# Second MLP product of nine blocks by seven sums, with the split first weights kept in DRAM

## The chip, the cores and the metric

One core of a Trainium2 chip. The metric is the device time of the whole program in microseconds (us). The granted TensorE clock was 1.00 in every stretch of the profile shown below.

## The reference

Attention with normalised queries and keys, then two MLPs of a model width of 768 and a hidden width of 3072, over 4 batches of 448 positions, all in fp32:

```python
x = attention(rmsnorm(q), rmsnorm(k), v)             # (4, 448, 768)
xn = (x - mean(x)) / sqrt(var(x) + 1e-06) * g_ln
x = x + maximum(xn @ w_ch1a, 0.0) @ w_ch2a           # first MLP
u = x + (x.transpose(0, 2, 1) @ U @ V).transpose(0, 2, 1)
out = u + maximum(u @ w_ch1b, 0.0) @ w_ch2b          # second MLP
```

## The kernel before

**Stages.** After the attention the MLP work is four stages `s`: stages 0 and 1 are the first MLP for the batches 0, 1 and 2, 3, stages 2 and 3 the second MLP. A stage has six blocks `j`. A block makes 512 hidden rows as two groups `g` (products of kind `G`, with `w1`), and then multiplies them with `w2` (products of kind `M`), adding to `acc`.

**Kind G.** A 2 by 2 block product made from seven products (`P1` to `P7`, order `ORDER`) of sums of inputs and of weights. The sums of the inputs (`in_hi`, `in_lo`) are made once for a stage, the sums of the weights once for a group by GpSimd (`weight_sum`, into `w_s1`, `w_s2`, or in place). VectorE puts the seven results together (`combine`), in the tiles `t_u2`, `t_c22`, `t_c12`, `t_c21`.

**Kind M.** Plain: 12 products a block (`OUTS`: six rows of output `d`, two halves), each for both batches and two chunks. After the second half VectorE adds two banks to `acc` (`gather`), twelve additions a block.

**Splitting.** Every operand is split into a high part in fp32r and a low part. ScalarE makes the high part (`weight_high`, `hidden_high`), VectorE subtracts to get the low one (`weight_low`, `hidden_low`), and TensorE makes three passes, high by high, high by low and low by high. So a `G` product is 3 chunks by 3 passes = 9 matmuls, an `M` product 2 x 2 x 3 = 12. A block has 14 x 9 + 12 x 12 = 270 matmuls, all 128x128 by 448 columns.

**Order.** `prods` is a list of all products. Every engine walks the same list, each at its own pace, and position `n` of the walk is product `n`. On VectorE a position is, in this order: a step of `mixing` where there is one, `weight_low` for the product 3 positions on, `hidden_low` or `make_low`, and last `combine` or `gather` of product `n`, which waits for that product. The split weights lie in a ring of 8 slots. A product's bank of PSUM (six of them) is given back when it has been read out. SyncE issues all DMAs, in the order of its own walk.

**Mixing.** In stages 1 and 2 twelve items of the step from the first to the second MLP (`U`, `V`) are run between products. An item begins every `MIX_STEP` = 22 positions. Its step for chunk `i` is: TensorE transposes at offset 4 + 3i, ScalarE `xs_hi` at 5 + 3i, VectorE `xs_lo` at 6 + 3i, and TensorE waits for that `xs_lo` at 7 + 3i. At offset 19 TensorE waits for what VectorE does at 18, and at 20 VectorE adds to `xa` twice.

Of the kernel before, what the change touches and what calls it, by code (L numbers as in the profile page):

```python
# [5 lines left out]
F32 = mybir.dt.float32  # L6
# [23 lines left out]
def mixer_kernel(nc, qkv, q_t, g_qk2, g_ln, u_lr, v_lr, w1, w2, out_t):  # L30
# [8 lines left out]
    STAGES = B  # L39
    assert D * 2 == P and KC == HC and NG == 2 * NJ and DC == 6 and B == 4  # L40
    xres = nc.dram_tensor("xres", (B, DC, P, S), F32).ap()
    xnrm = nc.dram_tensor("xnrm", (B, DC, P, S), F32).ap()


    prods = []
    for s in range(STAGES):
        for j in range(NJ):
            for g in (2 * j, 2 * j + 1):
                prods += [("G", s, g, k) for k in ORDER]
            prods += [("M", s, j, n) for n in range(len(OUTS))]  # L50
# [6 lines left out]
    def j_no(q):  # L57
        return prods[q][1] * NJ + prods[q][2]
# [5 lines left out]
    for q, (kind, s, n, k) in enumerate(prods):  # L64
# [3 lines left out]
        if kind == "M" and OUTS[k][1]:  # L68
            onto = number[kind, s, n, OUTS.index((OUTS[k][0], 0))]
        if onto is not None:  # L70
            banks[q] = banks[onto]
            before[q] = [onto]
        else:
            banks[q] = [free.pop(0) for _ in range(1 if kind == "G" else 2)]
            before[q] = [last_use.get(b) for b in banks[q]]
        if kind == "G" and k in LAST_IN_BANK or kind == "M" and OUTS[k][1]:
# [6 lines left out]
    for q in range(Q):  # L83
        kind, _, _, k = prods[q]
        if k == 0 or kind == "M" and k == 6:
            runs.append([])
        runs[-1].append(q)
        run_of.append(len(runs) - 1)
    high_at, low_at, sums_at, reload_at = {}, {}, {}, {}
    for r, run in enumerate(runs):  # L90
        for q in run:
            high_at.setdefault(q - 4, []).append(q)
            low_at.setdefault(q - 3, []).append(q)
        if prods[run[0]][0] == "G":
            for k, at in ((P5, -5), (P7, -5), (P6, -4), (P3, 0)):
                sums_at.setdefault(run[0] + at, []).append((r, k))
        reload_at.setdefault(run[-1] - 2, []).append(r)
    sum_no = {}
    for at in sorted(sums_at):
        for what in sums_at[at]:  # L100
            sum_no[what] = len(sum_no)
# [4 lines left out]
    def group_run_before(r):  # L106
        return next((n for n in range(r - 1, -1, -1) if prods[runs[n][0]][0] == "G"), None)

    RING = 8


    store_at = {}
    for s in range(STAGES):
        for d in range(DC):
            store_at[number["M", s, NJ - 1, OUTS.index((d, 1))] + 2] = s, d
# [32 lines left out]
    MIX_FROM, MIX_STEP, ITEMS = 4, 22, 2 * HC  # L148

    def mix_of(q):  # L150
# [3 lines left out]
        m, off = divmod(q - number["G", s, 0, 0] - MIX_FROM, MIX_STEP)  # L154
# [18 lines left out]
    with ExitStack() as ctx:  # L173
# [86 lines left out]
        w_in = [sem(f"w_in{i}") for i in range(2)]  # L260
        make_in = [[sem(f"make_in{c}_{n}") for n in range(4)] for c in range(HC)]
# [122 lines left out]
        def outs_done(s, j, d):  # L384
            return 12 * (s * NJ + j) + 2 * (d + 1)


        def read_out(eng, q, n=0):
            kind, s, j, k = prods[q]
            if kind == "M":  # L390
                eng.wait_ge(ev_done, outs_done(s, j, OUTS[k][0]) - 1 + n)
            elif k == P1:
                eng.wait_ge(p1_done, g_no(q) + 1)
            elif k == P2:
                eng.wait_ge(hlo_done, cut(g_no(q), C11))
            else:
                eng.wait_ge(comb_done, 5 * g_no(q) + COMB[k])


        def ended(q):  # L400
            return g_no(q) if 0 <= q < Q and prods[q][0] == "G" and prods[q][3] == P4 else None

        with nc.Block() as block:
            @block.sync
            def _(sp):
# [16 lines left out]
                def load_weights(r):  # L422
                    if r >= len(runs):
                        return
                    if r >= 2:
                        sp.wait_ge(wlo_done, runs[r - 2][-1] + 1)
                    kind, s, n, k = prods[runs[r][0]]
                    src = w1[s // 2, n].rearrange("p a c -> p (a c)") if kind == "G" else w2[s // 2, n, k // 6]
                    sp.dma_start(w_raw[r % 2][:].rearrange("p a c -> p (a c)"), src).then_inc(w_in[r % 2], 16)

                def load_made(s, c, n):
# [7 lines left out]
                    else:  # L439
# [6 lines left out]
                        if c == 2:  # L446
                            sp.wait_ge(hlo_done, 4 * NG * s)
# [34 lines left out]
                for what, n in seq:  # L482
# [17 lines left out]
                    if what != "step":  # L500
# [3 lines left out]
                        for r in reload_at.get(n, ()):  # L504
                            load_weights(r + 2)
# [759 lines left out]
```

## Time and profile before

| | |
|---|---|
| time, median of 3 runs | 1702.59 us (1702.48 to 1703.29) |
| time of the profiled execution | 1701.09 us, with a span of 1699.2 us |
| TensorE (PE) busy | 1660.1 us of the span, 98% |
| VectorE (DVE) busy | 1093.7 us, 64% |
| ScalarE (ACT) busy | 703.5 us, 41% |
| GpSimd (POOL) busy | 484.7 us, 29% |
| HBM traffic | 122.75 MB read, 24.77 MB written |

The span is cut into 40 equal slices in the profile. The first eight or so are attention; the MLP stages follow, from about 344 us to the end. A matmul's duration in the profile overlaps with that of the next one, so durations of matmuls are not added up. The lines (L772 and so on) are those of the kernel printed above.

### The profile page before, as it was taken

Reading aid. Unit: us, or ns where it says so; the run is one execution under the profiler, and the core shown is the slowest. Engines: PE = TensorE matmul, PEld = TensorE weight load, DVE = VectorE, ACT = ScalarE, POOL = GpSimd, SP = SyncE. Lnnn points to the kernel's source line nnn. Section 1 sums busy time; section 2 is a strip of 40 time slices with the busy share of each in tenths; the row PEclk is TensorE's granted clock in tenths of the full one; section 3 lists DMA queues with packets and bytes.
Section 4 is the critical chain, followed back from the end, with each engine's and each line's share of the span. In section 5 each row is a group of like instructions: output and inputs, shape, how many; then the busy total and the mean of one; then the engine's idle time right before and its main releaser. Section 6 shows DMA issues by size and latency. Waiting matters only on the chain.

```text
span 1699.2 us, 27419 instructions
## 1 busy us (share of the span) xinstructions
PE 1660.1 (98%) x10040; PEld 1481.5 (87%) x10040; DVE 1093.7 (64%) x2072; ACT 703.5 (41%) x1648; POOL 484.7 (29%) x434
## 2 busy tenths in 40 slices
PE   9989988999999999999999999999999999999999
PEld 7766666688999999999999999999999999999998
DVE  6887788856455659665556496655554966455654
ACT  5778888843233324332233243323322432223321
POOL 5666777621101114211111142110111321111110
PEclk9999999999999999999999999999999999999999
DMA  4222334222121124422222145222211441111112
GB/s 123 77 77 83 94 109 126 67 97 65 62 80 62 56 73 156 146 78 78 78 78 76 42 168 177 77 65 90 80 51 66 165 172 50 62 57 57 56 56 84
DMA packets 54867, 149.29 MB, mean 88 GB/s; under 512 B 6000, under 2 KB 36848, under 8 KB 54736
## 3 DMA queue, kind: packets, MB, share of 16 engines
q1 hardware_dynamic: 54736, 147.55, 26.6%
q8 instruction: 82, 1.34, 0.3%
q14 instruction: 49, 0.40, 0.1%
HBM read 122.75 MB, written 24.77 MB: 87 GB/s over the span
## 4 chain that ended last, share of the span: by engine, by line
PE 81%; DVE 1%; ACT 1%; issue 0%; DVEq 0%; ACTq 0%
PE mm_ps L772 41%; PE mm_ps L762 36%; PE mm_ps L719 1%; PE sc_ps L784 1%; PE sc_ps L794 1%; PE sc_ps L706 1%; PE mm_ps L698 1%; PE sc_ps L740 0%; PE sc_ps L802 0%; ACT e_t L871 0%; DVE h_lo L1102 0%; PE sc_ps L728 0%; ACT e_nat L859 0%; DVE x_nat L1015 0%; DVE mm_ps L1036 0%
## 5 line engine op out<-in xcount | busy, mean ns | idle before, releaser
L772 PE MATMUL mm_ps<-h_hi,w_hi 128*128 128x448 f32 x1152 | 423.2, 367 | 0.0
L772 PE MATMUL mm_ps<-h_hi,w_lo 128*128 128x448 f32 x1152 | 421.1, 366 | 0.0
L772 PE MATMUL mm_ps<-h_lo,w_hi 128*128 128x448 f32 x1152 | 421.1, 366 | 0.0
L1135 DVE TENSOR_TENSOR acc<-mm_ps,acc 128x448 f32<-128x448 f32 x288 | 166.1, 618 | 362.8 <-PE mm_ps L772 362.8
L762 PE MATMUL mm_ps<-in_hi,w_hi 128*128 128x448 f32 x1008 | 371.4, 368 | 0.0
L762 PE MATMUL mm_ps<-in_hi,w_lo 128*128 128x448 f32 x1008 | 368.4, 365 | 0.0
L762 PE MATMUL mm_ps<-in_lo,w_hi 128*128 128x448 f32 x1008 | 368.3, 365 | 0.0
L909 ACT ACTIVATE w_hi<-w_raw 128x256 fp32r<-128x256 f32 (+1 forms) x480 | 204.6, 452 | 189.3 <-PE mm_ps L772 168.4
L772 PEld LDWEIGHTS mm_ps<-h_hi,w_lo 128*128 128x128 f32 x1152 | 216.4, 188 | 17.7
L772 PEld LDWEIGHTS mm_ps<-h_lo,w_hi 128*128 128x128 f32 x1152 | 216.5, 188 | 17.2
L772 PEld LDWEIGHTS mm_ps<-h_hi,w_hi 128*128 128x128 f32 x1152 | 216.4, 188 | 17.1
L1089 DVE TENSOR_TENSOR w_lo<-w_raw,w_hi 128x256 fp32r<-128x256 f32 (+1 forms) x480 | 228.9, 489 | 0.6 <-ACT w_hi L909 0.3
L943 ACT ACTIVATE h_hi<-ht 128x448 fp32r<-128x448 f32 x144 | 83.4, 579 | 289.1 <-DVE ht L1120 155.7
L762 PEld LDWEIGHTS mm_ps<-in_hi,w_lo 128*128 128x128 f32 x1008 | 189.3, 188 | 15.5
L762 PEld LDWEIGHTS mm_ps<-in_lo,w_hi 128*128 128x128 f32 x1008 | 189.5, 188 | 14.7
L762 PEld LDWEIGHTS mm_ps<-in_hi,w_hi 128*128 128x128 f32 x1008 | 189.4, 188 | 14.6
L623 POOL TENSOR_TENSOR w_s<-w_raw,w_s 128x384 f32<-128x384 f32 x48 | 50.8, 1058 | 510.4 <-DVE w_lo L1089 510.4
L623 POOL TENSOR_TENSOR w_s<-w_raw 128x384 f32<-128x384 f32 x48 | 56.9, 1186 | 476.4 <-DMA w_raw<-in_w 407.1
L859 ACT ACTIVATE e_nat<-mm_ps,nbias,rs 112x448 f32<-112x448 f32 x192 | 137.1, 722 | 12.6 <-DVE nbias L1042 12.3
L1102 DVE SCALAR_TENSOR_TENSOR h_lo<-ht,h_hi 128x448 fp32r<-128x448 f32 x144 | 109.0, 757 | 32.2 <-ACT h_hi L943 32.1
L909 ACT ACTIVATE w_hi<-w_s 128x384 fp32r<-128x384 f32 x144 | 73.9, 516 | 116.1 <-POOL w_s L623 68.7
L1036 DVE TENSOR_REDUCE mm_ps<-mm_ps 112x2 f32<-112x896 f32 x96 | 104.8, 1092 | 17.8 <-PE mm_ps L698 17.3
(105 smaller groups left out, 1960.1 us busy)
## 6 DMA issues: line engine op xcount, KB each, us to landing
w_raw<-in_w SPq DMA_DIRECT2D x96, 768.0 KB, 4.4
qk<-in_qkv SPq DMA_DIRECT2D x23, 448.0 KB, 4.2
acc<-xres SPq DMA_DIRECT2D x6, 1344.0 KB, 9.4
qt_raw<-in_q_t SPq DMA_DIRECT2D x24, 224.0 KB, 3.1
v<-in_qkv SPq DMA_DIRECT2D x24, 224.0 KB, 2.6
xnrm<-st_n SPq DMA_DIRECT2D x24, 224.0 KB, 2.0
xres<-acc SPq DMA_DIRECT2D x24, 224.0 KB, 2.2
xa<-xres SPq DMA_DIRECT2D x24, 224.0 KB, 2.7
```

The source lines that it names most:

```text
L623: nc.gpsimd.tensor_tensor(out, in0, in1, op).then_inc(sum_done, 1)
L698: last = nc.tensor.matmul(mm_ps[:TP, 2 * (n % 2) + h, :S], a[rows, t % 2, i * TP:(i + 1) * TP], b[rows, t % 2], start=a is q_hi and b is k ...
L706: last = nc.tensor.transpose(to[:TP, c * TP:(c + 1) * TP], e_nat[:, n % 3, h, c * TP:(c + 1) * TP], ident[:TP, :TP])
L762: last = nc.tensor.matmul(bank(q), w[a][:, c * P:(c + 1) * P], x[:, k, c], start=k not in ONTO and c == 0 and p == 0, stop=c == HC - 1 and ...
L772: last = nc.tensor.matmul(bank(q, b), w[a][:, c * P:(c + 1) * P], x[:, half, 2 * c + b], start=half == 0 and c == 0 and p == 0, stop=half ...
L859: nc.scalar.activation(e_nat[:, n % 3, h], mm_ps[:TP, 2 * (n % 2) + h, :S], ACT.Exp, bias=nbias[:, n % 2, h:h + 1], scale=rs[:, t % 2, 0, ...
L909: nc.scalar.activation(w_hi[:, q % RING, :width(q)], weights(q), ACT.Copy).then_inc(whi_done, 1)
L943: nc.scalar.activation(h_hi[:, g % 2, h], src, ACT.Relu).then_inc(hhi_done, 1)
L1036: nc.vector.reduce_max(nmax(n), mm_ps[:TP, 2 * (n % 2):2 * (n % 2) + 2, :S], axis=AX, negate=True).then_inc(max_done, 1)
L1089: nc.vector.tensor_tensor(w_lo[:, q % RING, :w], weights(q), w_hi[:, q % RING, :w].bitcast(F32), ALU.subtract).then_inc(wlo_done, 1)
L1102: nc.vector.scalar_tensor_tensor(h_lo[:, g % 2, h], src, 0.0, h_hi[:, g % 2, h].bitcast(F32), ALU.max, ALU.subtract).then_inc(hlo_done, 1)
L1135: nc.vector.tensor_tensor(acc[:, b, d], bank(q, b), acc[:, b, d], ALU.add).then_inc(ev_done, 1)
```

## The change

Nine blocks change the form of their second product: `j` = 1 to 4 of stage 1 and `j` = 1 to 5 of stage 3. There the kind is `S`: seven products for each of three output chunks `d`, 21 products of 2 chunks by 3 passes = 6 matmuls, thus 126 matmuls for 144. The block has 252 matmuls for 270.

- **Activations.** ScalarE writes the rectified hidden rows plain (`hidden_relu`, 8 a block, into the tiles `make_a` and `make_b`), VectorE makes 8 differences of them (`hidden_sum`), ScalarE makes 14 high parts (`form_high`) and VectorE 14 low parts (`form_low`), where there were 8 `hidden_high` and 8 `hidden_low`.
- **w2.** GpSimd makes 12 sums of 128x256, ScalarE and VectorE split 21 weights of 128x256 (before 12). A low part is made 4 positions ahead of its product.
- **Read-out.** 21 additions to `acc` a block (before 12), one after each `S` product. A later product of the chain goes on top of the same bank.
- **w1.** In stages 0 and 2 the split weights of the groups of blocks 1 to 5 are stored to a DRAM tensor `w_kept` (high and low part, 384 KB a product, 140 stores). Stages 1 and 3 load them from there (140 loads, issued 7 positions ahead into the ring) and make neither sums nor splits for them; 20 loads of `w1` go away.
- **Mixing.** In stage 1 an item begins every 26 positions.

```diff
+BY_SUMS = (P1, P5, P6, P3, P7, P2, P4)
+SUMMED_ONTO = {P6: P1, P7: P6, P4: P7, P3: P5}
...
+    def by_sums(s, j):
+        return s % 2 == 1 and FIRST_KEPT <= j and (s == STAGES - 1 or j < NJ - 1)
...
+            if by_sums(s, j):
+                prods += [("S", s, j, (k, d)) for k in BY_SUMS for d in range(HC)]
...
+    def kept(q):
+        kind, s, n, _ = prods[q]
+        return kind == "G" and s % 2 == 1 and n // 2 >= FIRST_KEPT
...
+            fetch_at.setdefault(q - RING + 1, []).append(q)
...
+        high_at.setdefault(q - (5 if kind == "S" else 4), []).append(q)
+        low_at.setdefault(q - (4 if kind == "S" else 3), []).append(q)
...
+        if kind == "S" and k[0] in (P5, P7, P6, P3):
+            sums_at.setdefault(q - {P5: 9, P7: 8, P6: 6, P3: 6}[k[0]], []).append(q)
...
+            g1, m0 = number["G", s, 2 * j + 1, P1], number["S", s, j, (P1, 0)]
+            for k, m, sub, cut in (
+                    (P1, 0, None, g1 - 2), (P1, 1, None, g1), (P5, 0, g1 - 1, g1 + 1), (P5, 1, g1, g1 + 2),
+                    (P6, 1, g1 + 4, g1 + 5), (P3, 1, None, g1 + 6), (P6, 0, g1 + 6, m0), (P3, 0, None, m0 + 1),
+                    (P7, 1, m0 + 1, m0 + 4), (P7, 0, m0 + 2, m0 + 5), (P2, 0, None, m0 + 7), (P2, 1, None, m0 + 8),
+                    (P4, 1, m0 + 7, m0 + 11), (P4, 0, m0 + 8, m0 + 12)):
...
-    MIX_FROM, MIX_STEP, ITEMS = 4, 22, 2 * HC
+    MIX_FROM, MIX_STEP, ITEMS = 4, {1: 26, 2: 22}, 2 * HC
...
+                def load_split(q):
+                    _, s, g, k = prods[q]
+                    old = number["G", s - 1, g, k]
+                    slot_free(sp, q)
+                    sp.wait_ge(kept_out[old % RING], 16 * store_no[old])
...
+                        if k == P6:
+                            split(pool, number["S", s, n, (P5, d)])
+                            out, in0, in1, op = w, w, a11, ALU.subtract
+                        if k == P3:
+                            split(pool, number["S", s, n, (P6, d)])
+                            out, in0, in1, op = w, a12, w, ALU.subtract
...
+                def form_low(s, j, k, m):
+                    dve.wait_ge(hhi_done, cut_no["f", s, j, k, m])
+                    nc.vector.tensor_tensor(form(h_lo, k, m), form_tile(s, j, k, m), form(h_hi, k, m).bitcast(F32),
+                                            ALU.subtract).then_inc(hlo_done, 1)
...
+                    if kind == "S":
+                        b, d = ADDED_TO[k[0]][0], HC * ADDED_TO[k[0]][1] + k[1]
+                        dve.wait_ge(prod_done, q + 1)
+                        dve.wait_ge(ev_done, added_before[q])
+                        nc.vector.tensor_tensor(acc[:, b, d], bank(q), acc[:, b, d], ALU.add).then_inc(ev_done, 1)
+                        return
```

In that table `m0` is the first `S` product of the block and `g1` the first product of its second group; the third entry is the position of the difference on VectorE, the fourth that of the split on ScalarE and VectorE.

## Rows read from the trace of the kernel before

**Rows 1.** The page, chain that ended last, by engine.

```profile
PE 81%; DVE 1%; ACT 1%; issue 0%; DVEq 0%; ACTq 0%
```

**Rows 2.** Busy time in a 100 us window of stage 3 (x instructions), clock, DMA share, GB/s.

```profile
1390.00:1490.00 100.00, 100.00 (x495) 92.68 (x494) 53.76 (x100) 28.29 (x62) 16.58 (x16) 1.00 0.17 57
```

**Rows 3.** The chain in order of time, 1600 us to the end (start, us, what).

```profile
1611.08 29.19 PE mm_ps L772 x144
1640.26 25.53 PE mm_ps L762 x126
```

**Rows 4.** Groups by shape: busy us, mean ns, idle before.

```profile
L1089 DVE TENSOR_TENSOR w_lo<-w_raw,w_hi 128x256 fp32r<-128x256 f32 x288 | 124.3, 447 | 0.2
L1102 DVE SCALAR_TENSOR_TENSOR h_lo<-ht,h_hi 128x448 fp32r<-128x448 f32 x144 | 109.0, 757 | 32.2 <-ACT h_hi L943 32.1
L1089 DVE TENSOR_TENSOR w_lo<-w_s,w_hi 128x384 fp32r<-128x384 f32 x144 | 93.2, 647 | 0.1
L943 ACT ACTIVATE h_hi<-ht 128x448 fp32r<-128x448 f32 x144 | 83.4, 579 | 289.1 <-DVE ht L1120 155.7 <-DVE ht L1122 72.9 <-DVE ht L1124 60.5
```

**Rows 5.** DVE in order of time, end of a second group, stage 3.

```profile
1446.40 0.62 DVE L1102 SCALAR_TENSOR_TENSOR h_lo<-ht,h_hi 128x448 fp32r<-128x448 f32 x1 [0.32 <-ACT h_hi L943]
1446.95 0.62 DVE L1124 TENSOR_TENSOR ht<-mm_ps,ht 128x448 f32<-128x448 f32 x1
1447.49 0.42 DVE L1089 TENSOR_TENSOR w_lo<-w_raw,w_hi 128x256 fp32r<-128x256 f32 x1
1448.22 0.62 DVE L1102 SCALAR_TENSOR_TENSOR h_lo<-ht,h_hi 128x448 fp32r<-128x448 f32 x1 [0.31 <-ACT h_hi L943]
1448.77 1.09 DVE L1089 TENSOR_TENSOR w_lo<-w_raw,w_hi 128x256 fp32r<-128x256 f32 x3
```

**Rows 6.** PE in order of time, first matmul of a second product.

```profile
1446.75 0.37 PE L772 MATMUL mm_ps<-h_hi,w_hi 128*128 128x448 f32 x1
```

**Rows 7.** DVE and POOL in order of time, round a weight sum.

```profile
1422.96 0.55 DVE L1089 TENSOR_TENSOR w_lo<-w_raw,w_hi 128x384 fp32r<-128x384 f32 x1
1423.43 1.38 DVE L1089 TENSOR_TENSOR w_lo<-w_s,w_hi 128x384 fp32r<-128x384 f32 x1
...
1423.19 1.21 POOL L623 TENSOR_TENSOR w_s<-w_raw 128x384 f32<-128x384 f32 x1 [3.37 <-DVE w_lo L1089]
```

**Rows 8.** Single lines from 480 us on: ns min/median/max, first and last start.

```profile
L1089 DVE TENSOR_TENSOR w_lo<-w_s,w_hi x126: 541/548/1379, 511.7 to 1656.2; 128x384 fp32r<-128x384 f32 x126
L1102 DVE SCALAR_TENSOR_TENSOR h_lo<-ht,h_hi x129: 609/625/1577, 481.7 to 1667.1; 128x448 fp32r<-128x448 f32 x129
L1135 DVE TENSOR_TENSOR acc<-mm_ps,acc x264: 606/615/626, 495.6 to 1695.6; 128x448 f32<-128x448 f32 x132
L623 POOL TENSOR_TENSOR w_raw<-w_raw x42: 1007/1020/1219, 494.1 to 1643.4; 128x384 f32<-128x384 f32 x42
```

**Rows 9.** Other GpSimd shapes, whole span, the same columns.

```profile
L601 POOL TENSOR_TENSOR make<-make x12: 1125/1139/1605, 238.2 to 319.1; 128x448 f32<-128x448 f32 x12
L551 POOL TENSOR_TENSOR qk_sq<-qk x23: 1887/1893/2270, 11.1 to 315.3; 112x1024 f32<-112x1024 f32 x23
```

**Rows 10.** A mixing step on PE, and one on DVE.

```profile
705.50 0.28 PE L784 MATMUL sc_ps<-xs_hi,u_st 112*128 112x256 f32 x1
...
705.88 0.45 PE L772 MATMUL mm_ps<-h_hi,w_hi 128*128 128x448 f32 x1
...
719.95 0.41 DVE L1141 TENSOR_TENSOR xs_lo<-sc_ps,xs_hi 112x256 fp32r<-112x256 f32 x1
```

**Rows 11.** DMA: issues (count, KB, us to landing), and a 2 us window.

```profile
w_raw<-in_w SPq DMA_DIRECT2D x96, 768.0 KB, 4.4
...
1380.00:1382.00 2.00, 2.00 (x12) 1.85 (x11) 1.82 (x4) 1.03 (x3) 0.00 (x0) 1.00 1.05 403
```

**Rows 12.** The end: all engines, in order of time.

```profile
1695.02 1.16 DVE L1135 TENSOR_TENSOR acc<-mm_ps,acc 128x448 f32<-128x448 f32 x2 [3.71 <-PE mm_ps L772]
1696.21 0.81 SPq L466 DMA_DIRECT2D out<-acc  x2
```

More of the change, by code:

```diff
@@ L39, in mixer_kernel @@
     STAGES = B
+    FIRST_KEPT = 1
     assert D * 2 == P and KC == HC and NG == 2 * NJ and DC == 6 and B == 4
@@ L83, in mixer_kernel @@
     for q in range(Q):
[L84 to L97, printed above, removed]
+        kind, s, n, k = prods[q]
@@ new lines, in mixer_kernel @@
+    for at in sums_at:
+        if prods[sums_at[at][0]][0] == "G":
+            sums_at[at].sort(key=lambda q: (P5, P7, P6, P3).index(prods[q][3]))
+    for r, run in enumerate(runs[2:], 2):
+        kind, s, n, k = prods[run[0]]
+        if kind != "G" and s % 2 == 1 and n >= FIRST_KEPT:
+            at = number["G", s, 2 * n, P4 if run[0] in (number.get(("S", s, n, (P5, 0))), number.get(("M", s, n, 6))) else P5]
+        else:
+            at = runs[r - 2][-1] - 2
+        load_at.setdefault(at, []).append(r)
@@ L98, in mixer_kernel, with sums_before @@
     sum_no = {}
     for at in sorted(sums_at):
-        for what in sums_at[at]:
-            sum_no[what] = len(sum_no)
+        for q in sums_at[at]:
+            sum_no[q] = len(sum_no) + 1
     def product_of(r, k):
         return runs[r][ORDER.index(k)]
[L106 to L112, printed above, removed]
-    for s in range(STAGES):
-        for d in range(DC):
-            store_at[number["M", s, NJ - 1, OUTS.index((d, 1))] + 2] = s, d
+    def sums_before(q):
+        _, s, n, _ = prods[q]
+        first = number["S", s, n, (P1, 0)] if prods[q][0] == "S" else number["G", s, n, P1]
+        return next((x for x in range(first - 1, -1, -1) if x in sum_no
+                     and (prods[x][3] if prods[x][0] == "G" else prods[x][3][0]) == P3), None)
@@ L118, in mixer_kernel @@
+    relu_no, sub_no, cut_no = {}, {}, {}
+    for ats, nos in ((relu_at, relu_no), (sub_at, sub_no), (cut_at, cut_no)):
+        for at in sorted(ats):
+            for what in ats[at]:
+                nos[what] = len(nos) + 1
     N = NP_ * NI
@@ L764, in product @@
                                                         stop=c == HC - 1 and p == 2, skip_group_check=k in ONTO)
+                    elif kind == "S":
+                        k, d = k
+                        if d == 0:
+                            for m in range(2):
+                                cut(pe, "f", s, n, k, m)
+                        for m in range(2):
+                            for p, (a, x) in enumerate(((0, h_hi), (0, h_lo), (1, h_hi))):
+                                last = nc.tensor.matmul(bank(q), w[a][:, m * P:(m + 1) * P], form(x, k, m),
+                                                        start=k not in SUMMED_ONTO and m == 0 and p == 0,
+                                                        stop=m == 1 and p == 2, skip_group_check=k in SUMMED_ONTO)
                     else:
```

345 lines of the change are left out of this document (259 added, 86 removed).

## The prediction

> **What bounds the kernel.** I read the chain that ended last first: TensorE is 81% of the span of it [rows 1], and what is left is mostly attention. Then a window of stage 3: TensorE is busy all of it, VectorE for 54%, ScalarE for 28%, GpSimd for 17% [rows 2]. So in the MLP a matmul less is time gained, at the step from one matmul to the next, not at its duration (366 ns, which overlaps). The chain in order of time gives the step: 144 matmuls of one block's second product in 29.19 us, 0.2027 us each [rows 3]. That makes a `G` product 1.82 us, an `M` product 2.43 us, and the new `S` product 6 x 0.2027 = 1.216 us.
>
> **The gain.** 9 blocks x 18 matmuls x 0.2027 us = 32.8 us, 3.65 us a block, if TensorE never waits. Whether it waits is the whole question, since VectorE's 54% is a mean over a light and a heavy part.
>
> **VectorE's unit costs.** Steps, again, are shorter than durations when work is queued: 448 columns step by 0.545 us (1446.40 to 1446.95, to 1447.49), a `w_lo` of 128x256 by (1.09 - 0.42) / 2 = 0.335 us [rows 5]. I use 0.34 and 0.545 for all new operations too, since the fp32 kinds of before, from PSUM or from SBUF, have the same medians (615 and 625 ns, [rows 8]).
>
> **VectorE's load in an `S` stretch.** 21 products take TensorE 25.5 us. In them VectorE does 17 low parts of weights (the last four positions make none, because the next group's are loaded) = 5.8 us, 21 additions, 8 `form_low` and 4 `hidden_sum` = 33 x 0.545 = 18.0 us. Together 23.8 us of 25.5: it fits as a mean, with nothing over. In the group stretch it is light (no splits of `w1`), but it cannot work ahead, since each position ends in a wait for its own product.
>
> **Where in the stretch.** VectorE may fall behind by what the lead covers: product q needs the `w_lo` made at the start of position q - 4. Let T0 be the first `S` matmul.
> - Position 0 is late. Before, the last `combine` began 0.20 us after the first matmul of the second product (1446.95 against 1446.75 [rows 5, 6]). Now the difference for P6 and the form of P3 stand ahead of it (the first waits for a rectification of 0.58 us [rows 4] that itself waits for the `combine` before): some 0.5 us later, its end at T0 + 1.3. Behind it on ScalarE the rectification and the high part (two steps, to T0 + 2.45), `form_low` for P6 (3.1), the addition: position 1 begins at T0 + 3.6.
> - Positions 1 to 8 hold 8 `w_lo`, 8 additions and 9 further operations: 2.7 + 4.4 + 4.9 = 12.0 us, where TensorE's eight products take 9.7 us. So position 9 begins at T0 + 15.5 and its `w_lo` is there at 15.95. TensorE wants it for product 13 at 13 x 1.216 = 15.8. Without any stall VectorE is late by 0.15 us a block: just enough. After position 9 it catches up.
>
> **GpSimd's lock.** Any stall in positions 1 to 8 thus goes straight to TensorE. Beside a weight sum a VectorE operation of two SBUF inputs waits for GpSimd's whole operation: the `w_lo` of 1423.43 took 1.38 us for 0.55, a stall of 0.83, beside a sum that began at 1423.19 and that had itself waited for the `w_lo` before [rows 7]; GpSimd gets its turn between two queued VectorE operations. Maxima of 1379 and 1577 ns say the same, while the additions from PSUM never exceed 626 ns [rows 8]. The Trainium skill (SBUF — State Buffer, "Who interferes with whom") states just that: a VectorE instruction with two SBUF inputs contends with a GpSimd one that reads SBUF, and the loser blocks fully. By this rule alone all eight sums could be lost in full, 6.4 us a block at 0.8 us each; by the rows a share of them.
>  A sum of 128x256 is not in the trace. From 1.007 us (384 columns) and 1.125 (448) it would be 0.77, from 1.887 (1024, 112 partitions) 0.83 [rows 8, 9]: I take 0.8. One that falls behind a running operation then costs 0.8 - 0.18 = 0.6 (0.83 of 1.01 in the row). Eight of the twelve sums of a block (P6 and P3, released by the `w_lo` of P5 and P6, and P7) fall in positions 1 to 6, beside 14 operations of two SBUF inputs. Walking them: at position 1 the P6 sum comes between the difference and `form_low` (0.6); at 2 and 3 it runs beside an addition and delays only the next `w_lo` (0.3, 0.4); at 4 and 5 one stands between `w_lo` and `form_low` and another ahead of the next `w_lo` (0.6 + 0.3 each). Sum 3.1 us. Bounds: below, nothing. In the middle, the rate of before: means over the unhindered values by 99 and 132 ns x 144 (647 over 548, 757 over 625) and by 27 ns x 288 (447 over 420) = 41 us [rows 4, 5, 8] for 192 weight sums, 0.21 us a sum, 1.7 us a block. Above, 8 x 0.62 = 5.0. I take 3.1, since operations of two SBUF inputs stand about twice as dense there as before.
>
> **Stage 3, five blocks.** TensorE waits 0.15 + 3.1 = 3.25 us a block for 3.65 gained: -0.4 x 5 = -2 us.
>
> **Stage 1, four blocks.** Here the mixing takes the lead away: TensorE at offset 7 waits for `xs_lo` at VectorE's position before (0.41 us [rows 10]), so there a lag of four positions is not allowed. Block 3 has its offsets 6, 9, 12, 15 at positions 4, 7, 10, 13. VectorE starts position 4 at 3.6 + 4.3 + 0.9 = 8.8 (three positions with 3 `w_lo`, 3 additions and 3 operations, and 0.9 of stalls), `xs_lo` is there at 9.3, TensorE would be at product 5 at 6.1: wait 3.2. In the same way, with 0.4 us for TensorE's own part of the mixing (705.50 to 705.88 [rows 10]), the next three come to 2.2, 1.1 and 0. Sum 6.6. Blocks 1, 2 and 4 (offsets 12, 15, 18; 20, 6; 12, 15, 18) come to 5.9, 7.7 and 5.5. As GpSimd can run in the shadow of the mixing's operations I take 1.0 off each: 5.6 + 4.9 + 6.7 + 4.5 = 21.7 against 4 x 3.65 = 14.6: +7 us. Without stalls by the lock the four come to 12.2: -2.4 us.
>
> **The rest.** The end: one addition and one store behind the last matmul, not two of each (1.16 us and 0.81 us [rows 12]): 0.54 + 0.4 = -0.9. ScalarE has 14 high parts and 9 weights of 256 columns more a block, 14 of 384 fewer, and was busy 28% [rows 2]: off the path. SyncE's 280 new DMAs: a load is due 7 products after it is issued, 8.5 us at least, for 384 KB; 768 KB land 4.4 us after issue, and the queue has moved 403 GB/s [rows 11]. The heaviest stretch asks for 393 KB per 1.216 us, 323 GB/s. In stages 0 and 2 stores come at one per 1.82 us, 216 GB/s, beside `w1` at 61, and the slot is wanted 7 products later. Hidden, at nothing; if a load is late, TensorE waits for it at once, and each us a block costs 10.
>
> **Sum.** -2 + 7 - 0.9 = +4 to +5 us on the profiled 1701.1 us, which is 1.5 below the median of the runs. On the median: 1707.4 us.
>
> **Rivals.**
> - **The lock costs little.** If VectorE's queued operations mostly keep their turn, the wait is not 3.1 but between 0 and 1.7 us a block. With 1.7: stage 3 (1.85 - 3.65) x 5 = -9.0, stage 1, between its two sums, 17.4 - 14.6 = +2.8, end -0.9: 1695.5. With 0: -17.5 - 2.4 - 0.9: 1681.8. For it: the 0.21 us a sum of before. Against it: the row where GpSimd gets in between. It decides the sign: below about 2.6 us a block the change gains, above it loses. 0.28.
> - **All hidden:** VectorE's lateness doesn't reach TensorE at all: 1702.6 - 32.8 - 0.9 = 1668.9. It would need position 9 at 15.4 in every block and the mixing unhindered. 0.05.
> - **Loads late** in place of VectorE: 1 us in each of the ten blocks loaded, on top of the sum, 1717. The 403 GB/s speak against it. 0.04.
> - My forecast, VectorE behind by lag and lock, between 1699 and 1722 (the upper bound of 5.0 gives +7.5 + 13.1 - 0.9): 0.63, of which 0.18 lies within 0.2% (3.4 us, about what a measurement of this kernel can tell from no change) and 0.45 above.
>  So faster 0.33, same 0.18, slower 0.49. The range goes from 1685, most of the rival's, to 1722. The likeliest case's own is 1699 to 1722.
>
> **What would show it.** Matmuls 10040 - 162 on TensorE. In stage 3, 252 matmuls of a block in 51.1 us without waits, 54 to 55 with them, the wait at the products of P3 and P7 (numbers 10 to 13) and ended by `w_lo`. In stage 1 waits before the matmuls of the mixing, ended by `xs_lo`, 4 to 7 us a block. Maxima of 1.2 to 1.4 us in `form_low` and `w_lo` of 128x256 beside sums of about 0.8 us. Group stretches free of waits and of `w1` splits. Wrong I would be most likely through the lock, by 2 us a block in either direction, 18 us in all; next through position 1, if it begins before 3.6.

## The result, and the profile after

The changed kernel took 1707.86 us (median of 11 runs, 1704.62 to 1711.04) against 1702.48 us for the kernel before (median of 11). The ratio is 1.0032, with a 95% interval of 1.0023 to 1.0042: slower by a third of a per cent, where the forecast was 1707.4 us. That the total came out so near is in good part luck: terms of opposite sign that were off met, and the parts below take them apart.

The page of the changed kernel: span, busy time by engine, the chain by engine, and the new DMAs.

```profile
span 1705.3 us, 28105 instructions
PE 1643.8 (96%) x9878; PEld 1451.4 (85%) x9878; DVE 1174.9 (69%) x2220; ACT 733.7 (43%) x1715; POOL 498.2 (29%) x462
...
PE 69%; DVE 9%; issue 2%; ACT 2%; DMA 1%; SPq 0%; DVEq 0%; ACTq 0%
...
w_kept<-w_hl SPq DMA_DIRECT2D x140, 384.0 KB, 6.4
w_hl<-w_kept SPq DMA_DIRECT2D x140, 384.0 KB, 4.0
```

TensorE has the 162 matmuls fewer (9878 for 10040) and is busy for 16 us less, and yet the span is 6.2 us longer: it now waits. Beside the 81% of [rows 1] the chain that ended last is TensorE's for 69% only, and VectorE has 9% of it.

I read the length of each stage from its first matmul in the trace to that of the next stage (in stage 3 to the end of the span):

| us | before | after | difference |
|---|---|---|---|
| up to stage 0 | 343.8 | 343.8 | 0.0 |
| stage 0 (stores split weights) | 335.2 | 337.7 | +2.4 |
| stage 1 (four blocks by sums, mixing) | 343.8 | 353.4 | +9.6 |
| stage 2 (stores, mixing) | 343.7 | 344.6 | +0.9 |
| stage 3 (five blocks by sums) | 332.7 | 325.9 | -6.8 |

**Stage 3.** The chain in order of time, two blocks of the changed kernel:

```profile
1434.33 23.73 PE mm_ps L957 x117
...
1477.80 9.99 PE mm_ps L967 x48
1487.79 23.73 PE mm_ps L957 x117
...
1531.25 10.01 PE mm_ps L967 x48
1541.26 23.72 PE mm_ps L957 x117
```

A block takes 1487.79 - 1434.33 = 53.46 us. Its 252 matmuls need 51.1 at the 0.2027 us a matmul of [rows 3], so 2.35 us of waits are left, all in the `S` stretch (27.9 us for 25.54), at products 9, 10, 12 and 13. Before, a block took 54.72. VectorE in that stretch, in order of time (T0, its first matmul, is at 1513.16):

```profile
1512.81 0.98 DVE L1350 TENSOR_TENSOR make_a<-make_b,make_a 128x448 f32<-128x448 f32 x1 [0.31 <-ACT make_b L1159]
...
1517.11 0.41 DVE L1316 TENSOR_TENSOR w_hl<-w_s,w_hl 128x256 fp32r<-128x256 f32 x1
1517.44 0.61 DVE L1350 TENSOR_TENSOR make_a<-make_b,make_a 128x448 f32<-128x448 f32 x1
1517.98 1.16 DVE L1354 TENSOR_TENSOR h_lo<-make_b,h_hi 128x448 fp32r<-128x448 f32 x1
...
1521.88 0.64 DVE L1316 TENSOR_TENSOR w_hl<-w_s,w_hl 128x256 fp32r<-128x256 f32 x1
1522.45 1.17 DVE L1354 TENSOR_TENSOR h_lo<-make_a,h_hi 128x448 fp32r<-128x448 f32 x1
...
1524.42 1.16 DVE L1354 TENSOR_TENSOR h_lo<-make_a,h_hi 128x448 fp32r<-128x448 f32 x1
...
1530.79 0.41 DVE L1316 TENSOR_TENSOR w_hl<-w_raw,w_hl 128x256 fp32r<-128x256 f32 x1
```

and GpSimd beside it:

```profile
1512.57 0.74 POOL L791 TENSOR_TENSOR w_s<-w_s,w_raw 128x256 f32<-128x256 f32 x1 [5.55 <-DVE w_hl L1316]
...
1517.60 1.05 POOL L791 TENSOR_TENSOR w_s<-w_s,w_raw 128x256 f32<-128x256 f32 x1 [1.59 <-DVE w_hl L1316]
...
1521.50 0.74 POOL L791 TENSOR_TENSOR w_s<-w_raw,w_s 128x256 f32<-128x256 f32 x1 [0.36 <-DVE w_hl L1316]
1522.20 0.93 POOL L791 TENSOR_TENSOR w_raw<-w_raw 128x256 f32<-128x256 f32 x1
1523.10 1.12 POOL L791 TENSOR_TENSOR w_s<-w_raw,w_s 128x256 f32<-128x256 f32 x1
1524.17 2.00 POOL L791 TENSOR_TENSOR w_raw<-w_raw 128x256 f32<-128x256 f32 x2
```

A `w_lo` is written as `w_hl` in the changed kernel, whose tile holds both parts. Position 1 begins with the one at 1517.11, T0 + 3.95. In the positions up to 9 three operations are 1.16 us long for 0.61 and one `w_lo` 0.64 for 0.41: stalls of 3 x 0.55 + 0.23 = 1.9 us, each beside a GpSimd sum. Position 9 begins with the `w_lo` at 1530.79, T0 + 17.6. It is ready at about T0 + 18.05, and TensorE wanted it at T0 + 15.8: 2.25 us late, which is the wait of the block. The difference at 1512.81, ahead of T0, is a fourth long one: 0.98 us for 0.61, beside the sum at 1512.57, a stall of 0.37. With it the stalls come to 2.25 us, the whole of the wait. GpSimd's row at 1517.60 shows the take-over: it is 1.05 us for an operation of 0.74, since it first waits for the difference at 1517.44 to end, and then holds back the `h_lo` of 1517.98.

**Stage 1.** Whom TensorE waited for in stage 1:

```profile
PE sc_ps L989 <- DVE xs_lo L1402: 10.5, 5, 3.0
PE mm_ps L967 <- DVE w_hl L1316: 1.8, 4, 0.6
```

The waits are at the mixing, as foreseen. But the matmuls behind a long one look odd. TensorE in order of time, block 1:

```profile
769.64 0.36 PE L967 MATMUL mm_ps<-h_hi,w_hl 128*128 128x448 f32 x1
772.75 0.58 PE L989 MATMUL sc_ps<-xs_hi,u_st 112*128 112x256 f32 x1 [2.76 <-DVE xs_lo L1402]
...
773.63 0.72 PE L967 MATMUL mm_ps<-h_hi,w_hl 128*128 128x448 f32 x1
774.15 0.57 PE L967 MATMUL mm_ps<-h_lo,w_hl 128*128 128x448 f32 x1
```

and the same stretch in 2 us windows (the third figure from the right is the granted clock):

```profile
768.00:770.00 2.00, 2.00 (x10) 1.50 (x9) 1.25 (x3) 2.00 (x6) 0.72 (x1) 1.00 0.00 0
770.00:772.00 2.00, 0.00 (x0) 0.00 (x0) 2.00 (x4) 0.48 (x2) 1.04 (x1) 1.00 0.00 0
772.00:774.00 2.00, 1.25 (x5) 1.25 (x6) 2.00 (x5) 0.00 (x0) 0.89 (x1) 0.68 0.00 0
774.00:776.00 2.00, 2.00 (x6) 1.76 (x6) 0.44 (x2) 1.87 (x5) 1.58 (x3) 0.50 0.00 0
776.00:778.00 2.00, 2.00 (x11) 1.82 (x10) 1.74 (x4) 0.17 (x1) 0.71 (x1) 0.97 0.00 0
```

TensorE stands still for 2.76 us, and just as it resumes the granted clock falls from 1.00 (2.4 GHz) to 0.50 (1.2 GHz) and comes back after 3.4 us; matmuls step by 0.37 us meanwhile (774.15 to 774.52 in the trace, where the next begins). That happens in blocks 1, 2 and 3, after waits of 2.76, 3.03 and 2.70 us, and not in block 4, where the longest wait is 1.37 us. At half clock for 3.4 us TensorE loses 1.7 us of work at most, 5.1 for the three. What they cost the stage is less, since TensorE would in part have waited for VectorE anyway: in experiment 9 none of the three came, and stage 1 took 350.4 us, 3.0 less (the `S` stretches of blocks 1, 2 and 3 took 0.5, 1.5 and 1.1 less). So about 3 us, a third of the stage's +9.6, go with the clock. The forecast had no term for it.

**Stages 0 and 2.** In the last block of stage 0 ScalarE stands for 2.78 us, the longest of its waits for a slot whose store has not landed:

```profile
641.92 0.53 ACT L1113 ACTIVATE w_hl<-w_s 128x384 fp32r<-128x384 f32 x1 [2.78 <-DMA w_kept<-w_hl]
```

SyncE's issues before it:

```profile
631.54 0.33 SPq L575 DMA_DIRECT2D w_raw<-in_w  x1
631.99 1.83 SPq L609 DMA_DIRECT2D make_a<-xnrm  x4
633.87 0.93 SPq L579 DMA_DIRECT2D w_kept<-w_hl  x2
634.91 3.75 SPq L609 DMA_DIRECT2D make_b<-xnrm  x4
638.71 3.65 SPq L579 DMA_DIRECT2D w_kept<-w_hl  x5
```

Only in this block do the loads for the next stage stand between the stores. The block takes 57.35 us for 54.72 before, the last of stage 2 takes 56.05 for 55.13. This differs from kernel to kernel: in the eight of the experiments that keep the order of the stores (1 to 6, 9 and 10) the two blocks together are 1.1 to 2.5 us longer than before, and part of that is the 2% slower stretches told of at the end.

### The profile page after: what moved, and what is told of

It is laid out like the page before. It is cut to its first block, busy times and chain, and to the rows that moved or that the text cites. A ratio compares the mean times of both kernels' runs of the same rounds, so it can differ in the third digit from the quotient of the medians.

```text
span 1705.3 us, 28105 instructions
## 1 busy us (share of the span) xinstructions
PE 1643.8 (96%) x9878; PEld 1451.4 (85%) x9878; DVE 1174.9 (69%) x2220; ACT 733.7 (43%) x1715; POOL 498.2 (29%) x462
## 4 chain that ended last, share of the span: by engine, by line
PE 69%; DVE 9%; issue 2%; ACT 2%; DMA 1%; SPq 0%; DVEq 0%; ACTq 0%
PE mm_ps L957 33%; PE mm_ps L977 26%; PE mm_ps L967 7%; DVE acc L1387 2%; DVE h_lo L1354 2%; DVE make_a L1350 2%; DVE w_hl L1316 1%; DMA w_kept<-w_hl 1%; PE mm_ps L911 1%; PE sc_ps L989 1%; PE sc_ps L898 1%; PE mm_ps L890 1%; PE sc_ps L999 1%; ACT h_hi L1171 0%; PE sc_ps L932 0%
## 5 line engine op out<-in xcount | busy, mean ns | idle before, releaser
L957 PE MATMUL mm_ps<-in_hi,w_hl 128*128 128x448 f32 x2016 | 586.8, 367 | 2.4 <-DVE ht L1375 2.4
L977 PE MATMUL mm_ps<-h_hi,w_hl 128*128 128x448 f32 x1440 | 416.6, 367 | 0.0
L957 PEld LDWEIGHTS mm_ps<-in_hi,w_hl 128*128 128x128 f32 x2016 | 378.6, 188 | 33.8 <-issue 3.1
L957 PE MATMUL mm_ps<-in_lo,w_hl 128*128 128x448 f32 x1008 | 368.5, 366 | 0.0
L977 PEld LDWEIGHTS mm_ps<-h_hi,w_hl 128*128 128x128 f32 x1440 | 270.4, 188 | 22.3
L977 PE MATMUL mm_ps<-h_lo,w_hl 128*128 128x448 f32 x720 | 263.3, 366 | 0.0
L967 PE MATMUL mm_ps<-h_hi,w_hl 128*128 128x448 f32 x756 | 229.9, 375 | 8.1 <-DVE w_hl L1316 7.6
L1113 ACT ACTIVATE w_hl<-w_raw 128x256 fp32r<-128x256 f32 (+1 forms) x400 | 166.6, 439 | 117.0 <-PE mm_ps L977 77.6
L957 PEld LDWEIGHTS mm_ps<-in_lo,w_hl 128*128 128x128 f32 x1008 | 189.4, 188 | 15.0
L1316 DVE TENSOR_TENSOR w_hl<-w_raw,w_hl 128x256 fp32r<-128x256 f32 (+1 forms) x400 | 187.7, 476 | 4.4 <-ACT w_hl L1113 4.2
L967 PEld LDWEIGHTS mm_ps<-h_hi,w_hl 128*128 128x128 f32 x756 | 144.3, 191 | 29.3 <-DVE w_hl L1316 17.7
L977 PEld LDWEIGHTS mm_ps<-h_lo,w_hl 128*128 128x128 f32 x720 | 135.3, 188 | 10.9
L967 PE MATMUL mm_ps<-h_lo,w_hl 128*128 128x448 f32 x378 | 139.6, 369 | 0.0
L1148 ACT ACTIVATE h_hi<-ht 128x448 fp32r<-128x448 f32 x90 | 52.1, 579 | 173.4 <-DVE ht L1375 91.0
```

The source lines that it names most:

```text
L957: last = nc.tensor.matmul(bank(q), w[a][:, c * P:(c + 1) * P], x[:, k, c], start=k not in ONTO and c == 0 and p == 0, stop=c == HC - 1 and ...
L967: last = nc.tensor.matmul(bank(q), w[a][:, m * P:(m + 1) * P], form(x, k, m), start=k not in SUMMED_ONTO and m == 0 and p == 0, stop=m == ...
L977: last = nc.tensor.matmul(bank(q, b), w[a][:, c * P:(c + 1) * P], x[:, half, 2 * c + b], start=half == 0 and c == 0 and p == 0, stop=half ...
L1113: nc.scalar.activation(w_hi[:, q % RING, :width(q)], weights(q), ACT.Copy).then_inc(whi_done, 1)
L1148: nc.scalar.activation(h_hi[:, g % 2, h], summed(g, h), ACT.Relu).then_inc(hhi_done, 1)
L1316: nc.vector.tensor_tensor(w_lo[:, q % RING, :w], weights(q), w_hi[:, q % RING, :w].bitcast(F32), ALU.subtract).then_inc(wlo_done, 1)
```

## The experiments

Each kernel is the changed one with the edit shown. Ratios are against the kernel before, with 95% intervals; blocks and stages are read from one profile each. The lengths of stages are given where the theories differ. The part up to stage 0, the same work in every kernel, took from 343.8 to 346.8 us in these profiles, so the spans of two profiles are compared by stage only. Two theories stood: VectorE's lag up to position 9 and GpSimd's lock set the wait (mine), or VectorE's load as a whole does.

**1. The lock taken away.**

```diff
-                        nc.gpsimd.tensor_tensor(out, in0, in1, op).then_inc(sum_done, 1)
+                        nc.gpsimd.tensor_tensor(out[:, :8], in0[:, :8], in1[:, :8], op).then_inc(sum_done, 1)
```

> Leaves work out: GpSimd's twelve sums of the second weights of an S block are made on 8 columns, not 256, so the output is not the reference's. All waits stay. Theory (VectorE falls behind by its lag at position 0 and by GpSimd's lock): the three stalls of 0.55 us and the one of 0.2 in positions 1 to 8 go, so a block of stage 3 falls from 53.46 us to about 51.6 (51.1 is the floor of 252 matmuls), 9 us in stage 3, and about 1.5 us a block in stage 1, 6 us: in all 15 us less than the changed kernel, a span of some 1690. Rival (the load of the stretch as such, the lock is a side matter): no more than 3 us less.

Measured 1689.33 us, 0.9925 (0.9908 to 0.9941). The low parts of stage 3, minimum, median and maximum in ns, in this kernel:

```profile
L1354 DVE TENSOR_TENSOR h_lo<-make_a,h_hi x40: 611/624/627, 1445.0 to 1678.2; 128x448 fp32r<-128x448 f32 x40
L1354 DVE TENSOR_TENSOR h_lo<-make_b,h_hi x30: 612/622/627, 1439.6 to 1673.7; 128x448 fp32r<-128x448 f32 x30
```

No stall is left, and an `S` stretch of stage 3 takes 25.65 us for 27.92: a block of 51.2, where 51.6 was expected. Position 1 now begins at T0 + 3.59 and position 9 at T0 + 15.35, so the stall ahead of T0 went too. Stage 1 fell by 6.0 to 347.5. VectorE has as many operations as in the changed kernel, and TensorE hardly waits in stage 3. So there it is the lock, and not the load alone. The Trainium skill (SBUF — State Buffer, "Who interferes with whom") states that a VectorE instruction with two SBUF inputs contends with a GpSimd one that reads SBUF. The traces agree: the stalls are those of operations with two SBUF inputs, while the additions from PSUM in stage 3 of the changed kernel never exceed 625 ns.

**2. Two operations out of positions 1 and 2.**

```diff
-                    (P7, 1, m0 + 1, m0 + 4), (P7, 0, m0 + 2, m0 + 5)
+                    (P7, 1, g1 + 5, m0 + 4), (P7, 0, m0, m0 + 5)
```

> The two differences for P7 are made at positions g1 + 5 and m0 instead of m0 + 1 and m0 + 2; nothing is left out. Theory (only what stands between position 0 and position 9 counts): the one goes to the light group stretch, the other fills VectorE's 0.84 us of idle time at position 0, so positions 1 and 2 are 1.09 us shorter and a block of stage 3 falls from 53.46 to about 52.4 us; stage 1 gains 0.8 a block; in all 8 us less than the changed kernel. Rival (VectorE's whole load over the stretch sets the time): no change, within 1 us.

Measured 1698.43 us, 0.9979 (0.9970 to 0.9988). The `S` stretches of stage 3 take 26.7 to 26.9 us for 27.92, 1.1 less, as worked out; stage 1 fell by 3.8. The same work in other positions is now a little faster than the kernel before. If VectorE's load over the block as a whole had counted, the time would not have moved.

**3. A wider mixing step.**

```diff
+    def pace(item):
+        return (4, 4) if item < ITEMS else (3, 0)
...
-                    i, part = divmod(off - 7, 3)
+                    wide, late = pace(item)
+                    i, part = divmod(off - 4 - wide, wide)
...
-                    if off == 18:
+                    if off == (21 if late else 18):
```

> In stage 1 a mixing step takes 4 positions instead of 3, and TensorE waits for a low part two positions behind VectorE instead of one; an item still fits in 26 positions. Nothing is left out. Theory (the mixing takes TensorE's lead away): TensorE's waits for xs_lo, some 26 us in all with those of the weight loads, lose about 1 us at each of the ten or so places; stage 1 falls from 353.4 to some 344 to 347 us, stage 3 stays at 53.46 a block. Rival (the wait only moves to the next w_lo, since VectorE's load is what counts): stage 1 gains less than 2 us.

Measured 1704.54 us, 1.0016 (1.0005 to 1.0027). Stage 1 fell by 2.9 to 350.6, between the two expectations. Whom TensorE waited for in stage 1 shows why it gained so little:

```profile
PE sc_ps L993 <- DVE xs_lo L1408: 7.0, 6, 1.7
PE sc_ps L1003 <- DMA xa<-xres: 5.1, 4, 2.2
```

The longest wait for `xs_lo` fell from 3.0 to 1.7 us, but an item now fills all 26 positions up to the next, and TensorE waits 5.1 us for the load of `xa`. The experiment brought in a wait of its own and settles nothing about size. Two falls of the clock came in it too, behind waits of 1.87 and 1.72 us.

**4. Sums in stage 3 alone.**

```diff
-        return s % 2 == 1 and FIRST_KEPT <= j and (s == STAGES - 1 or j < NJ - 1)
+        return s == STAGES - 1 and FIRST_KEPT <= j
...
-    MIX_FROM, MIX_STEP, ITEMS = 4, {1: 26, 2: 22}, 2 * HC
+    MIX_FROM, MIX_STEP, ITEMS = 4, {1: 22, 2: 22}, 2 * HC
```

> Only the five blocks of stage 3 go by sums; stage 1 has the plain M products (mixing items every 22 positions, as in the kernel before), while the split first weights are still loaded in both. Theory: stage 1 goes back to the 343.8 us of the kernel before (from 353.4), the rest stays, so 9.6 us less than the changed kernel, a span of 1695.7 and 3.4 us less than the kernel before, about 0.2% faster. Rival (the loads and stores of the split weights are what costs in stage 1, not VectorE): stage 1 stays above 348 us.

Measured 1699.36 us, 0.9986 (0.9977 to 0.9995). Stage 1 takes 344.7 us with its weights still loaded: the loads cost about 1 us there, the sums the rest.

**5. The mixing placed elsewhere.**

```diff
-    MIX_FROM, MIX_STEP, ITEMS = 4, {1: 26, 2: 22}, 2 * HC
+    MIX_AT, ITEMS = {1: (4, 26, 48, 81, 116, 150), 2: (4, 26, 48, 70, 92, 114)}, 2 * HC
```

> The six mixing items of stage 1 begin at positions 4, 26, 48, 81, 116 and 150 of the stage instead of every 26, each in 22 positions with its steps as in the changed kernel, so that but for one of them no wait of TensorE for xs_lo falls in positions 0 to 9 of an S stretch. Nothing is left out. Theory (the mixing takes the lead away just where VectorE lags): the S stretches of blocks 2, 3 and 4, 35.5, 33.9 and 29.6 us, come to about 29 each, as in stage 3 with TensorE's own part of the mixing; block 1 gains 1 to 2 us; stage 1 falls from 353.4 to about 342, some 11 us less in all. Rival (VectorE's extra operations for the mixing are what costs, wherever they stand): less than 4 us.

Measured 1716.23 us, 1.0082 (1.0067 to 1.0097): 8 us slower than the changed kernel, where 11 less were expected. Both expectations missed. TensorE's waits in stage 1:

```profile
PE sc_ps L990 <- DVE xs_lo L1403: 12.2, 4, 3.8
PE sc_ps L1000 <- DMA xa<-xres: 3.4, 1, 3.4
```

and the clock in block 2, behind the wait that ended at 848.6:

```profile
840.00:848.00 8.00, 4.66 (x22) 3.36 (x19) 8.00 (x18) 3.47 (x9) 0.36 (x1) 1.00 0.00 0
848.00:852.00 4.00, 3.43 (x12) 3.18 (x13) 2.34 (x7) 0.99 (x3) 0.00 (x0) 0.57 0.00 0
```

I had taken it that VectorE has caught up soon after position 9. It has not: a position with one `w_lo` and one addition takes it 0.88 us for TensorE's 1.216, so each wins back 0.33 us of a lag of up to four positions, and the first wait for `xs_lo`, now at product 12 or 13, pays the lag at once, 3.6 to 3.8 us in blocks 2, 3 and 4. Block 1 has one of 3.4 us for the load of `xa`. All four are followed, or in part covered, by 3.4 or (once) 6.8 us at half clock. In the changed kernel the one block whose first such wait is as late, block 2, has the longest, 3.03 us; blocks 3 and 4, with earlier ones, have 2.70 and 1.37 us at the longest.

**6. GpSimd's sums for P7 earlier.**

```diff
-            sums_at.setdefault(q - {P5: 9, P7: 8, P6: 6, P3: 6}[k[0]], []).append(q)
+            sums_at.setdefault(q - {P5: 9, P7: 17, P6: 6, P3: 6}[k[0]], []).append(q)
```

> GpSimd's three sums for P7 of an S block, which wait for no split, are made right behind those for P5, in the group stretch, instead of at positions 4 to 6 of the S stretch. Nothing is left out. Theory (a GpSimd sum costs a stall where VectorE has no slack): two of the three stalls of 0.55 us and part of the 0.2 are gone, a block of stage 3 falls from 53.46 to about 52.3 us, and in all some 8 us less than the changed kernel. Rival (GpSimd's next sum takes the place of the one moved and the stalls stay as many): less than 2 us.

Measured 1703.24 us, 1.0005 (0.9993 to 1.0016), 10 runs from 1697 to 1709. The `S` stretches of stage 3 take 26.8 us, 1.1 less: two stalls, as worked out. Stage 1 gained nothing (354.1). Its profile has 3.4 and 6.8 us at half clock in two places, and one wait of 2.28 us for a load of `xa`.

**7. The stores first.**

```diff
+                        if stored(n):
+                            store_split(n)
                         for s, c, tile in load_made_at.get((what, n), ()):
                             load_made(s, c, tile)
                         for what in store_at.get(n, ()):
                             store_acc(*what)
-                        if stored(n):
-                            store_split(n)
```

> SyncE issues the store of a split weight ahead of the loads for the next stage's inputs that stand at the same position, instead of behind them. Nothing is left out. Theory (in the last block of stages 0 and 2 a slot of the ring comes free late, since its store stands behind loads that wait): the last block of stage 0 goes from 57.35 to 54.7 us and that of stage 2 from 56.05 to 55.1, about 3 us less in all. Rival (the stores are late through the queue's traffic, not through the order of issue): no change, within 1 us.

The last block of stage 0 takes 54.72 us (57.35), that of stage 2 55.13 (56.05), both as in the kernel before: the order of issue is the cause. In experiments 8, 11 and 12, with the same order, the last block of stage 0 takes 54.72 us too. The time is 1706.22 us, 1.0026 (1.0015 to 1.0036), an interval that overlaps with that of the changed kernel; the gain of 3 us is that of one profile against one, and of the times no gain is clear.

**8. All four** (2, 5, 6 and 7 together).

> The differences for P7 early, the sums for P7 early, the mixing items placed and the stores first, all together; nothing is left out. Theory (the causes are separate and add): in stage 3 a block comes to about 51.3 us, 11 us less, stage 1 to about 335, 18 us less, the stores 3: a span of some 1674 to 1678, 1.3 to 1.5% faster than the kernel before. Rival (they are one cause counted four times, VectorE's load): no better than the best of them alone by more than 5 us, a span over 1688.

Measured 1687.49 us, 0.9919 (0.9905 to 0.9934). That misses the expected span of 1674 to 1678 us by some 10, and is at the edge of the rival's 1688. Stage 3 takes 319.4 us: its `S` stretches of 26.04 us are as long as its `G` stretches, so the waits are gone there, but both run 2% slower than 25.54, and a block takes 52.1 for the 51.3 expected. Stage 1, with the placing that had proved bad, takes 345.9, some 11 us over what was expected.

**9. TensorE kept busy while it waits.**

```diff
+                    if (item, off) in ((3, 7), (4, 7)):
+                        for _ in range(12):
+                            nc.tensor.matmul(sc_ps[1][:, S:S + 64], ident[:], ident[:, :64], start=True, stop=True)
```

> In two places of stage 1, before TensorE's wait for xs_lo in the S stretches of blocks 2 and 3 (3.0 and 2.7 us of wait in the changed kernel, each followed by some 3.3 us at a granted clock of 0.5), TensorE makes 12 small matmuls of 64 columns into unused columns of PSUM. The wait of 2.8 us in block 1 is left as it is. Nothing is left out, work is added. Theory (the stretches at half clock follow from TensorE standing still): the clock stays at 1.00 behind the two filled waits and falls behind the unfilled one; the S stretches of blocks 2 and 3 fall from 35.5 and 33.9 us to about 33.9 and 32.3, some 3 us in all. Rival (the clock falls for another reason, say the load of the whole stretch): all three drops stay and the time rises by what of the added matmuls is not hidden.

Measured 1705.77 us, 1.0020 (1.0011 to 1.0030). TensorE in order of time, block 2 (an `f32` matmul of `ident` shows as two), and windows round the unfilled wait of block 1 and the filled one of block 2:

```profile
848.05 2.79 PE L986 MATMUL sc_ps<-ident 128*128 128x64 f32 x24
851.27 0.38 PE L992 MATMUL sc_ps<-xs_hi,u_st 112*128 112x256 f32 x1 [0.43 <-DVE xs_lo L1405]
```

```profile
770.00:774.00 4.00, 1.20 (x8) 0.83 (x7) 4.00 (x9) 0.98 (x3) 1.43 (x2) 1.00 0.00 0
...
852.00:856.00 4.00, 4.00 (x23) 3.51 (x22) 2.87 (x8) 0.69 (x2) 0.00 (x0) 1.00 0.39 109
```

Behind both filled waits the clock stayed at 1.00, and the two `S` stretches fell by 1.5 and 1.1 us (35.50 to 34.04, 33.90 to 32.83), for matmuls that take the time of the wait. But this time it stayed at 1.00 behind the unfilled 2.8 us too, so the control did not come out as expected: the run agrees with the theory and does not prove it alone. Over the profiles of all these kernels stage 1 has nine waits of 3.0 us or more; none was without a fall of the clock. Of ten between 2.5 and 2.8 us four had one, and of fifteen between 1.4 and 2.3 us four. So a wait goes with a fall the more often the longer it is, and what decides in a single case stays open. The kernel before and the two with plain products in stage 1 have neither such waits nor a fall of the clock in stages 0 to 3 up to the last matmul.

**10. Low parts of the mixing one position earlier.**

```diff
-                    i, part = divmod(off - 6, 3)
+                    i, part = divmod(off - 5, 3)
...
-                    if off == 18:
+                    if off == 17:
```

> VectorE makes the low parts of the mixing one position earlier in its walk (at offset 5 + 3i and 17, where ScalarE makes the high ones), so TensorE waits for a low part two positions behind VectorE; TensorE's own steps stay where they are and an item still takes 22 of 26 positions. Nothing is left out. Theory (TensorE waits for VectorE's lag at the mixing, and long waits cost again through the clock): each wait is 1.2 to 1.5 us shorter, those of 2.7 to 3.0 us fall below 2 and with them the drops of the clock; stage 1 goes from 353.4 to 343 to 346 us, stage 3 stays. Rival (VectorE now waits for ScalarE and TensorE in turn, and the lag only grows): less than 3 us, with new idle time of VectorE before xs_lo.

Measured 1697.0 us, 0.9969 (0.9956 to 0.9981): 11 us less than the changed kernel. Stage 1 takes 345.0 us (353.4), and the longest wait for `xs_lo` is 1.8 us:

```profile
PE sc_ps L989 <- DVE xs_lo L1402: 6.5, 5, 1.8
```

One drop of the clock is left in stage 1, of three. That is what experiment 3 was to show, without a change to the load of `xa`.

**11. Stage 3 alone, with 2, 6 and 7.**

> Sums in the five blocks of stage 3 alone (stage 1 as plain M products with items every 22 positions), with the differences and the GpSimd sums for P7 early and the stores first; nothing is left out. Theory: stage 1 as before at 344, a block of stage 3 at 51.2 as the lock's and the lag's parts are both gone: 335 + 344 + 344 + 314 and the 344 ahead of them, a span of 1680 to 1684, about 1.1% faster than the kernel before. Rival (part of what all_four gained came from stage 1): over 1688.

Measured 1684.88 us, 0.9894 (0.9879 to 0.9909). A block of stage 3 takes 51.1 to 51.2 us, the floor of its matmuls, and the whole stage 314.1.

**12. All nine blocks, with 2, 6, 7 and 10.**

> Nine blocks by sums, with the differences and the GpSimd sums for P7 early, the stores first and the low parts of the mixing one position early; nothing is left out. Theory: stage 3 as in s3_best, stage 1 below the 343.8 us of the plain products for the first time, at 337 to 342, since no wait is long enough for the clock to fall: a span of 1674 to 1681, at or below s3_best. Rival (sums don't pay in a stage with mixing, however the steps stand): above s3_best by 2 us or more.

Measured 1676.31 us, 0.9842 (0.9827 to 0.9857): 1.6% faster than the kernel before and 1.8% than the changed one. Stage 1 takes 336.4 us, for the first time less than the 343.8 of plain products. Its window:

```profile
680.00:1020.00 340.00, 334.23 (x1675) 306.26 (x1674) 247.48 (x463) 125.56 (x293) 67.64 (x70) 1.00 0.46 156
```

TensorE is idle for 6 us of it, with the clock at 1.00 throughout. Of the 32.8 us that the matmuls left out are worth, this version gets 26.

## Why the prediction was right, and where it was not

- **The gain and its unit.** 0.2027 us a matmul and 32.8 us without waits hold: 25.59 us for 126 matmuls in the best version, 1.6% in all.
- **The likeliest case,** VectorE behind by lag and by GpSimd's lock, waited for at the `w_lo` of products 10 to 13 in stage 3 and at `xs_lo` in stage 1, is what the trace shows. Its parts:
  - Position 1 was put at T0 + 3.6 and is at 3.95. The 0.35 is a stall by the lock too, ahead of the positions that the forecast walked: without the lock (experiment 1) it is at 3.59, and position 9 at 15.35, for 15.5. So the lag alone was sized well.
  - The stalls were put at 3.1 us a block and are 1.9, or 2.25 with the one ahead of T0. A sum of 128x256 takes 0.74 us (0.8 taken) and costs 0.55 (0.6 taken): the unit was near. The count was high: three full stalls where I had three, but of the four short ones of 0.3 to 0.4 only one of 0.23 came, since most of these sums end in the shadow of an addition. Experiments 1, 2 and 6 confirm the mechanism, its place and its unit.
  - So the wait of a stage 3 block was put at 3.25 us and is 2.35, and stage 3 with the end came to -6.8 us, where -2 and -0.9 had been forecast.
- **Stage 1** was put at +7 and is +9.6. The waits alone came out near the 21.7 us taken, at some 22 (132.5 us in the four `S` stretches, less 102.2 of matmuls, about 3 of clock and 5.2 of TensorE's own mixing, which the same four stretches of the kernel before have too). That is luck in part: with 1.9 us of stalls the forecast's own arithmetic, between its two sums, gives 18. And the step had no term for the clock that falls behind the long waits, about 3 us. Experiments 10 and 12 bear out that the mixing takes the lead away. The step that VectorE catches up after position 9 was too easy a word; experiment 5, built on it, cost 8 us.
- **The DMAs at nothing** failed at one place: the stores are late in the last block of stages 0 and 2, +3.3 us in this profile (experiment 7), less in most others. The forecast weighed the queue's rate and the lead, and did not walk SyncE's list past the loads for the next stage, which is the work the stores are queued behind. The loads were never late for a matmul in the group stretches.
- **The sum** was +4 to +5 and is +6.2 in the profiled executions: stage 3 better by some 4 us, clock and stores worse by 6, the rest of stage 1 about as forecast. The total is right in part because these met. Its terms, -2 + 7 - 0.9, give +4.1 and 1706.7 us on the median; 1707.4 is the upper end of what was stated.

Of the rivals, "the lock costs little" set the break-even at 2.6 us of stalls a block. With 1.9 the forecast's own arithmetic would have given a gain of about 5 us. The lock as sized in the forecast thus did not decide the sign: the clock and the stores, 6 us together, and some 5 us of waits that this arithmetic doesn't have (the later position 1 in nine blocks is part of them) took it to the slower side. That the change came out slower, as forecast, is luck to that extent. "All hidden" and late loads did not occur.

## What to carry to other kernels

An engine at 69% of the span can still be the one that is waited for: walk its list position by position against the lead that its consumer has, and put work where it idles, not where its result is next wanted. Moving a few operations and issues, with nothing left out, turned 0.3% slower into 1.6% faster.

A wait in which the consumer is held one position behind its producer takes away the lead of everything else on that engine; give it two. A long wait of TensorE costs more than its length if the granted clock falls behind it, and here that happened after nine of nine waits of 3.0 us or more and after four of fifteen of 1.4 to 2.3 us: look at the clock in windows of a few us behind each wait.

Walk the list of the engine that issues the DMAs as well, and put the transfer that frees a buffer ahead of one that only prepares a later stage.

## What the runs showed of the hardware

- TensorE's granted clock fell to 0.50 for 3.4 us as it resumed from a wait (in a few places for 6.8 us; it began from 1.7 us before to 1.6 us after the wait's end): after 2.76, 3.03 and 2.70 us of wait in the changed kernel, after 1.65 us in one place of experiment 10, and not after 2.8 us in one place of experiment 9. Matmuls of 448 columns step by 0.37 us meanwhile, for 0.203.
- Such falls also come in the part up to stage 0, the same work in every kernel, in some profiles and not in others. It took 343.8 to 344.1 us in the four profiles without one, 345.2 to 346.0 in the seven with one of 3.4 us, and 346.5 to 346.8 in the three with two. So one cost 1.1 to 2.2 us there.
- Stretches of whole products ran 2% slower at a granted clock of 1.00: a group of 126 matmuls in 26.04 us for 25.53, in the chain of experiment 2:

```profile
1375.24 26.04 PE mm_ps L957 x126
1401.28 29.76 PE mm_ps L977 x144
```

  They fall on other blocks in each profile (none in stage 3 of the kernel before, nearly all of stage 3 in experiment 8). They may be why the times of the kernels with these DMAs spread more widely; that, and what causes them, was not tried.
- GpSimd's sums of two SBUF operands took 0.74 us at 256 columns and 0.20 at 8. A VectorE operation of two SBUF inputs beside one of 256 columns was held back by 0.23 to 0.55 us in stage 3 of the changed kernel.
